# Attention, a routed expert layer and a dense MLP in one kernel: MLP tiles in a new order, rows added up behind each expert, narrower gate products

## The chip, the core and the metric

The kernel runs on one core of one Trainium2 chip. The metric is device time in microseconds (us) of one execution, the median of several. The engines of the core run side by side, each through its own instruction list, and wait for each other through semaphores: TensorE (PE, with its weight loads shown apart as PEld), VectorE (DVE), ScalarE (ACT), GpSimd (POOL) and SyncE (SP, which here only issues DMAs).

## What is computed

Three layers, one behind the other, on 2 x 768 = 1536 tokens of width 512, all in float32:

```python
# 1. attention, 2 x 8 heads of 64, with 4 sink keys and a window of 128
keep = is_sink | in_window
a = softmax(where(keep, q @ k.T / 8, -1e9)); x = a @ v          # -> x: (1536, 512)
# 2. routed experts: tokens with x @ w_skip > 0 go to one of 8 experts
e_idx = argmax(x @ w_gate); gate_w = softmax(x @ w_gate)[e_idx]
out = x.copy()
out[active] = x + gate_w * (relu(x @ w1[e]) @ w2[e])           # w1: (8, 512, 1024)
# 3. dense MLP on every token: 512 -> 2048 -> 512
h = out @ w_in
g = where(h > 0, h, exp(min(h, 0)) - 1)
return g @ w_out
```

With the drawn inputs 653 of the 1536 tokens are active. Their counts by expert are 69, 177, 98, 15, 21, 114, 89 and 70. Of the first 1152 tokens (nine tiles of 128) 561 have no expert.

## The kernel before

**Attention.** Head pairs are worked through in 48 units of 128 queries. TensorE makes the scores (`qk`, line 1280), turns the probabilities (`turn_unit`, 1306), and multiplies by the values (`pv`, 1350). Every second unit it turns the finished columns of `x` (`turn_x`, 1322) and multiplies them by the gate weights (`gate`, 1332). The gate weights `wg` are 9 columns wide (8 experts and the skip score) but stand in a tile of 119 columns, the rest zero (memset in line 663), and the product is made over all 119. The finished rows lie in `x_tok` in SBUF and are stored to `tokens_dram` (line 587).

**Routing** (lines 1121 to 1181 on VectorE, 1421 to 1454 on TensorE). From the scores each active token gets a slot: the experts follow each other in chunks of 128 slots, each expert padded to a whole chunk. Which token stands in which slot is found by small bf16 products: `here` is a 0/1 tile of token against row, made for 12 token tiles, first for chunk 0 alone and then for all chunks; the sums give `sources`, the list of token rows that each chunk gathers. `slot_i` is the reverse: the slot of each token; a token without an expert points past the slots to a row of zeros.

**Experts.** Nine chunks run here (one expert has two). GpSimd gathers a chunk's 128 rows from `tokens_dram` into `xg` by an indirect DMA (`gather_chunk`, lines 696 to 709); the gather of chunk k may start when TensorE has turned chunk k-1 out of `xg` (`xg_turned`). On TensorE a chunk is 64 matrix records of up products (`ps_h`, 1470), the turn of the *next* chunk into `ps_x` (4 records, 1439), and 24 down products (`ps_y`, 1259). ScalarE rounds `h` to its high part (843), copies `ps_x` to `xg_t` (837) and splits the weights to come into high and low halves (476 and 480; the low halves by VectorE, 484 and 489). VectorE copies `ps_y` to `y_sb` (1194), and ScalarE issues its store to `slots_dram` (848).

**From the experts to the MLP.** When the last store has landed, GpSimd gathers the slots of token tiles 0, 1 and 2 into `row_sb` (line 742). VectorE scales each by its gate and adds `x_tok` (`combine`, line 1214). TensorE turns it (1489), ScalarE and VectorE make `x_hi` (868) and `x_lo` (1221), and then the first up product of the MLP may start.

**MLP.** Four blocks of three token tiles, each with 16 steps of 12 up products (`ps_g`, 1259) and 9 down products (`ps_out`, 1514); up products run one step ahead of the activation. The next block's tiles are gathered, combined and turned behind it. SyncE stores `out` tile by tile (637), and GpSimd gathers the next tile into the same buffer after that. SyncE loads the last three weight pieces only behind the first gather of tile 2 (line 630).

The order that matters for the last chunk is, on VectorE and GpSimd:

```python
1192                dve.wait_ge(down_done, g + 2)
...
1194                dve.tensor_copy(y_sb[:], ps_y[:]).then_inc(y_copied, 1)
...
731            pool.wait_ge(y_stored, end * 16 + 16)
...
1213                dve.wait_ge(gathered[i], tb * 16 + 16)
```

Of the kernel before, what the change touches and what calls it, by code (L numbers as in the profile page):

```python
# [16 lines left out]
HOT = 6  # L17
BIG = 3.0e38
# [3 lines left out]
def build(nc, q_t, k_s, v_p, n_sink, window, w_skip, w_gate, w1, w2, w_in, w_out, out):  # L22
# [40 lines left out]
    GW = P - E1  # L63
    DV = DH + 1
    PV = 2 * DV
    assert PC == DC and 2 * DH == P and QT == 2 * PG and 4 * SK == P
# [22 lines left out]
    slots_dram = nc.dram_tensor("slots", [SLOTS + 2 * P, D], F32, kind="Internal").ap()  # L89

    tokens_dram = nc.dram_tensor("tokens", [N + P, D], F32, kind="Internal").ap()
    token_tiles = tokens_dram.rearrange("(t p) d -> p t d", p=P)
    slot_chunks = slots_dram.rearrange("(c p) d -> c p d", p=P)
# [15 lines left out]
    with ExitStack() as ctx:  # L109
# [22 lines left out]
        x_tok = sb("x_tok", [P, NT, D])  # L132
        identity = sb("identity", [P, P])
        gates = sb("gates", [P, NT])
        slot_i = sb("slot_i", [P, NT], I32)
# [9 lines left out]
        with ExitStack() as routing:  # L145
            scope.append(routing)
            wg = sb("wg", [P, DC, GW])
            zeros = sb("zeros", [P, D])
            token_f = sb("token_f", [P, 2, NT])
            scores = sb("scores", [P, NT, E1])  # L150
# [112 lines left out]

        with ExitStack() as experts:
            scope.append(experts)
            xg = sb("xg", [P, D])
# [10 lines left out]
            y_sb = sb("y_sb", [P, D])  # L277
            ps_h = [psum(f"ps_h{i}", [P, KP, P]) for i in range(2)]
            ps_x = psum("ps_x", [P, DC, P])
            ps_y = psum("ps_y", [P, D])  # L280
            ps_source = psum("ps_source", [P, 512])
            scope.pop()


        with ExitStack() as mlp:
            scope.append(mlp)
            x_hi = sb("x_hi", [P, DC, TW], F32R)
            x_lo = sb("x_lo", [P, DC, TW], F32R)
# [7 lines left out]
            row_sb = [sb(f"row_sb{i}", [P, D]) for i in range(TB)]  # L296
            ps_g = [psum(f"ps_g{i}", [P, 512]) for i in range(2)]
            ps_out = [psum(f"ps_out{i}", [P, D]) for i in range(TB)]
            ps_x2 = [psum(f"ps_x2{i}", [P, DC, P]) for i in range(TB)]
# [14 lines left out]
        gate_padded = sem("gate_padded")  # L314
# [62 lines left out]

        xg_loaded = sem("xg_loaded")
# [11 lines left out]
        combined = sem("combined")  # L390
# [140 lines left out]
        def _(sp):  # L531
# [42 lines left out]
            def zero_slots(third):  # L574

                if third == 0:
                    sp.wait_ge(zeros_set, 2)
                    sp.dma_start(tokens_dram[N:, :], zeros[:]).then_inc(tokens_stored, 16)
                every = slots_dram.rearrange("(c p) d -> p c d", p=P)
                first, end = (CHUNKS + 2) * third // 3, (CHUNKS + 2) * (third + 1) // 3  # L580
# [53 lines left out]
            with sp.Fori(0, NB) as tb:  # L634
                for i in range(TB):
                    sp.wait_ge(out_copied, tb * TB + i + 1)
                    sp.dma_start(out_tiles[bass.ds(tb * TB + i, 1)].rearrange("o p d -> (o p) d"),
                                 row_sb[i][:]).then_inc(out_stored[i], 16)
            for i in range(TB):
                sp.wait_ge(out_stored[i], 16 * NB)  # L640

        @block.gpsimd
        def _(pool):
# [19 lines left out]
            pool.memset(wg[:, :, E1:GW], 0.0).then_inc(gate_padded, 1)  # L663
# [8 lines left out]
            iota(chunk_at[:, 0, :], [[P, CHUNKS + 1]])  # L672
            iota(rel[:], [[1, S]], by_partition=-1)
# [3 lines left out]
            pool.wait_ge(iotas_done, 15)  # L677
# [5 lines left out]
            pool.memset(sources[:], N).then_inc(const_done, 1)  # L683
# [12 lines left out]
            def gather_chunk(k):  # L696
                if not (isinstance(k, int) and k == 0):

                    pool.wait_ge(xg_turned, k)
                pool.tensor_copy(source_i[:], sources[:, bass.ds(k, 1)]).then_inc(source_picked, 1)  # L700
                pool.wait_ge(source_picked, k + 1)
                if not (isinstance(k, int) and k == 0):
# [3 lines left out]
                    out=xg[:], out_offset=None, in_=tokens_dram[:, :],  # L706
                    in_offset=bass.IndirectOffsetOnAxis(ap=source_i[:], axis=0),
                    bounds_check=N, oob_is_err=False,
# [8 lines left out]
            gather_chunk(1)  # L717

            for e in range(E):
                first, hi = bases  # L720

                gather_chunk(first + 2)
                with pool.If(first + 1 < hi):
                    with pool.Fori(first + 1, hi) as g:
                        gather_chunk(g + 2)
# [3 lines left out]


            pool.wait_ge(y_stored, end * 16 + 16)
            pool.wait_ge(xg_loaded, end * 16 + 32)
            pool.wait_ge(xg_copied, end + 1)
            pool.wait_ge(idle_done, end + 2)
            pool.tensor_tensor(idle[:], idle[:], idle[:], ALU.subtract).then_inc(idle_done, 1)
            for t in range(NT):

                if t >= 2 * TB:
                    pool.wait_ge(out_stored[t % TB], 16 * (t // TB - 1))
                elif t >= TB:  # L740
                    pool.wait_ge(x2_turned, t - TB + 1)
                pool.indirect_dma_start(
                    out=row_sb[t % TB][:], out_offset=None, in_=slots_dram[:, :],
                    in_offset=bass.IndirectOffsetOnAxis(ap=slot_i[:, t:t + 1], axis=0),
                    bounds_check=SLOTS, oob_is_err=False,
                ).then_inc(gathered[t % TB], 16)

        @block.scalar
        def _(act):
# [89 lines left out]
            def chunk(g, hook):  # L839
                for i in range(2):  # L840
# [6 lines left out]
                act.wait_ge(y_copied, g + 2)  # L847
                act.dma_start(slot_chunks[bass.ds(g, 1)].rearrange("o p d -> (o p) d"),
                              y_sb[:]).then_inc(y_stored, 16)
# [755 lines left out]
```

## Time and profile before

| | us |
|---|---|
| median of 3 runs | 572.84 |
| lowest, highest | 571.85, 573.89 |
| the profiled execution | 572.68 |
| its span, first to last instruction | 570.7 |
| TensorE busy | 536.2 (94%) |
| VectorE, ScalarE, GpSimd busy | 273.4, 211.4, 43.5 |

The stages in the span: attention to about 142, routing to 157, experts to 278, the change-over to 293, the MLP to the end. All times in the text are from the start of the span. In the profile a TensorE record's "busy" holds its latency; how fast a run of products is, is read from the chain or from the distance of two starts. PEclk is the granted TensorE clock as a share of 2.4 GHz: 1.00 is 2.4 and 0.50 is 1.2.

### The profile page before, as it was taken

The page shows a single profiled execution, that of the slowest core. Times are in us where ns is not written, and L with a number is a line of the kernel's source. Part 1 is how long each engine was busy: PE and PEld are TensorE (multiplying, and loading weights), DVE is VectorE, ACT ScalarE, POOL GpSimd, SP SyncE. Part 2 cuts the span into 40 slices and gives each one's busy share as a digit, 9 for nine tenths or more (in the row PEclk, how much of TensorE's full clock was granted, in tenths as well). Part 3 has the DMA queues.
Part 4 walks back from the last instruction along what each step waited for, and adds up shares of the span by engine and source line. Part 5 has one row for each costly group of instructions (what it writes and reads, how often), then busy time and mean ns, then how long its engine had stood idle before and what let it go on. Part 6 is the DMA issues. An engine that isn't in the chain of part 4 may idle for free.

```text
span 570.7 us, 8866 instructions
## 1 busy us (share of the span) xinstructions
PE 536.2 (94%) x3211; PEld 466.3 (82%) x3212; DVE 273.4 (48%) x706; ACT 211.4 (37%) x419; POOL 43.5 (8%) x98
## 2 busy tenths in 40 slices
PE   5999999998599999999579999999999999999997
PEld 3777777777399999999468999898998989999986
DVE  7565655553744144458436663433443344433332
ACT  3575655553033133346214532422233222332222
POOL 6000000000110000100220000010002000000000
PEclk9999999999589999999859999999999999999999
DMA  9288897322029759999472000110003000010001
GB/s 211 73 291 289 262 310 271 113 94 109 23 77 332 259 179 357 354 344 373 152 241 75 2 0 1 57 55 1 0 1 92 18 1 0 0 56 0 1 0 56
DMA packets 47943, 73.21 MB, mean 128 GB/s; under 512 B 16484, under 2 KB 16740, under 8 KB 47908
## 3 DMA queue, kind: packets, MB, share of 16 engines
q1 hardware_dynamic: 43570, 64.23, 33.0%
q0 software_dynamic: 1840, 6.03, 3.5%
q10 hardware_dynamic: 2498, 2.51, 1.3%
q8 instruction: 19, 0.31, 0.2%
q14 instruction: 16, 0.13, 0.1%
HBM read 58.08 MB, written 14.68 MB: 128 GB/s over the span
## 4 chain that ended last, share of the span: by engine, by line
PE 91%; DVE 4%; issue 2%; DMA 2%; ACT 1%; POOL 0%; DVEq 0%; POOLq 0%; ACTq 0%
PE ps_g L1259 24%; PE ps_out L1514 23%; PE ps_h L1470 12%; PE ps_y L1259 9%; PE ps_pv L1350 7%; PE ps_qk L1280 5%; PE ps_turn L1306 4%; PE ps_turn L1332 2%; PE ps_pv L1362 1%; DVE prob L974 1%; PE ps_x L1489 1%; PE ps_x L1439 1%; PE ps_turn L1314 1%; DMA row_sb<-slots,slot_i 1%; DMA xg<-tokens,source_i 1%
## 5 line engine op out<-in xcount | busy, mean ns | idle before, releaser
L1259 PE MATMUL ps_g<-x_hi,w_hi 128*128 128x384 f32 x256 | 87.6, 342 | 1.5 <-DVE x_lo L1221 1.5
L1259 PE MATMUL ps_g<-x_lo,w_hi 128*128 128x384 f32 x256 | 87.1, 340 | 0.0
L1259 PE MATMUL ps_g<-x_hi,w_lo 128*128 128x384 f32 x256 | 87.1, 340 | 0.0
L887 ACT ACTIVATE g_raw<-ps_g 128x384 f32<-128x384 f32 x64 | 31.5, 492 | 129.6 <-PE ps_g L1259 129.5
L1229 DVE TENSOR_SCALAR g_raw<-g_raw 128x384 f32<-128x384 f32 x64 | 23.1, 361 | 116.2 <-ACT g_raw L887 112.0
L1514 PE MATMUL ps_out<-w_hi,g_lo 128*128 128x512 f32 x192 | 75.8, 395 | 0.0
L1514 PE MATMUL ps_out<-w_lo,g_hi 128*128 128x512 f32 x192 | 75.6, 394 | 0.0
L1514 PE MATMUL ps_out<-w_hi,g_hi 128*128 128x512 f32 x192 | 75.5, 393 | 0.0
L1470 PEld LDWEIGHTS ps_h<-xg_t,up_w 128*128 128x128 f32 x576 | 67.7, 197 | 2.0 <-issue 1.3
L1470 PE MATMUL ps_h<-xg_t,up_w 128*128 128x128 f32 x576 | 67.9, 280 | 0.9 <-ACT xg_t L837 0.9
L891 ACT ACTIVATE g_hi<-g_raw 128x384 fp32r<-128x384 f32 x64 | 33.7, 526 | 62.3 <-DVE g_raw L1232 62.3
L1237 DVE TENSOR_TENSOR g_lo<-g_raw,g_hi 128x384 fp32r<-128x384 f32 x64 | 35.7, 558 | 36.1 <-ACT g_hi L891 36.1
L1259 PEld LDWEIGHTS ps_g<-x_hi,w_hi 128*128 128x128 f32 x256 | 49.0, 191 | 4.4 <-issue 1.9
L1259 PEld LDWEIGHTS ps_g<-x_hi,w_lo 128*128 128x128 f32 x256 | 49.0, 191 | 2.6
L1350 PE MATMUL ps_pv<-v_pad,prob_t 128*128 128x130 f32 x352 | 49.5, 282 | 0.0
L1259 PEld LDWEIGHTS ps_g<-x_lo,w_hi 128*128 128x128 f32 x256 | 48.9, 191 | 0.0
L762 ACT ACTIVATE prob<-prob,low 128x288 f32<-128x288 f32 (+1 forms) x96 | 43.6, 504 | 13.5 <-DVE low L974 13.2
L1350 PEld LDWEIGHTS ps_pv<-v_pad,prob_t 128*128 128x128 f32 x352 | 43.7, 193 | 4.2 <-ACT prob_t L776 4.2
L974 DVE CUSTOM_DVE_ANT_0 prob<-ps_qk,bias 128x288 f32<-128x288 f32 (+1 forms) x96 | 38.5, 421 | 13.1 <-PE ps_qk L1280 12.3
L1514 PEld LDWEIGHTS ps_out<-w_hi,g_lo 128*128 128x128 f32 x192 | 36.0, 188 | 8.3
L1514 PEld LDWEIGHTS ps_out<-w_hi,g_hi 128*128 128x128 f32 x192 | 36.0, 188 | 6.2 <-ACT g_hi L891 0.5
L1514 PEld LDWEIGHTS ps_out<-w_lo,g_hi 128*128 128x128 f32 x192 | 36.0, 188 | 6.0
(144 smaller groups left out, 688.0 us busy)
## 6 DMA issues: line engine op xcount, KB each, us to landing
raw<-in_moe_w SPq DMA_DIRECT2D x16, 1024.0 KB, 7.0
up_w<-in_moe_w SPq DMA_DIRECT2D x16, 1024.0 KB
raw<-in_moe_w_in SPq DMA_DIRECT2D x4, 1024.0 KB, 7.1
raw<-in_moe_w_out SPq DMA_DIRECT2D x4, 1024.0 KB, 6.1
slots<-zeros SPq DMA_DIRECT2D x2, 1792.0 KB, 9.5
v_pad<-in_v SPq DMA_DIRECT2D x16, 192.0 KB, 4.8
tokens<-x_tok SPq DMA_DIRECT2D x6, 512.0 KB, 4.5
out_tokens<-row_sb SPq DMA_DIRECT2D x12, 256.0 KB, 2.1
```

The lines of the kernel that those rows point to most:

```text
L762: act.activation(out_, out_, ACT.Exp, bias=low[:, n % 4:n % 4 + 1], scale=-1.0).then_inc(prob_ready, 1)
L887: act.activation(g_raw[f % GB][:], ps_g[f % 2][:, 0:TW], ACT.Exp).then_inc(g_exp_done, 1)
L891: act.activation(g_hi[f % GB][:], g_raw[f % GB][:], ACT.Copy).then_inc(g_hi_done, 1)
L974: dve.tensor_tensor_reduce(out=prob_of(u, h), in0=ps_qk[n % 4][:, 0:w], in1=bias_of(u % QT), scale=-SCALE, scalar=BIG, op0=ALU.add, op1=AL ...
L1229: dve.tensor_scalar(g_raw[f % GB][:], g_raw[f % GB][:], 1.0, 1.0, ALU.min, ALU.subtract).then_inc(g_min_done, 1)
L1237: dve.tensor_tensor(g_lo[f % GB][:], g_raw[f % GB][:], g_hi[f % GB][:], ALU.subtract).then_inc(g_lo_done, 1)
L1259: last = pe.matmul(to, w, x, start=start and m == 0, stop=stop and m == 2)
L1280: pe.matmul(ps_qk[(2 * u + h) % 4][:, 0:w], q_pair[p % 2][rows, i * P:(i + 1) * P], k_pair[p % 2][rows, first:first + w], start=True, stop ...
L1306: last = pe.transpose(ps_turn[h][:, m, :], prob_of(u, h)[:, c:c + P], identity[:])
L1350: last = pe.matmul(ps_pv[g % 2][:, u % 2 * PV:(u % 2 + 1) * PV], prob_t[u % 2][:, h, m, :], v_pad[p % 2][h][:, tile, :], start=(u % 2 == 0 ...
L1470: last = pe.matmul(ps_h[i][:, f, :], up_w[half][i][:, c, f * P:(f + 1) * P], xg_t[:, c, :], start=(c == 0), stop=(c == DC - 1))
L1514: return pe.matmul(ps_out[i][:], act[f % GB][:, i * P:(i + 1) * P], weight, start=(f == 0 and act is g_hi and weight is high), stop=(f == ...
```

## The change

Six things change together.

1. **Order of the MLP.** The tokens of the first nine tiles (`ET` = 9) are sorted: those without an expert first, then by expert. Tiles 9 to 11 keep their order. New work on VectorE (4 operations ahead of the chunk lists, then `place_tokens`: 11 small operations, 9 of 128 columns, 1 copy) and on TensorE (18 products into `ps_place` in the routing, 18 into `ps_list` behind the first expert) makes `lists`: for each place of the nine tiles the row to gather and the row of `out` to write.
2. **One table of rows.** Slots and tokens lie in one DRAM tensor `rows`; a token without an expert is gathered from its token row. The zero rows behind the slots are gone.
3. **Rows are finished in the experts.** ScalarE copies `xg` to `x_keep` (two buffers in turn) behind `xg_t`; VectorE's copy of `ps_y` becomes `ps_y * gate + x_keep`. The gates by slot come from 12 bf16 products of 60 columns (`sum_gates`), which stand behind the first chunk's up products. `combine` is gone, and `x_tok` is no longer kept.
4. **Gathers.** `gather_chunk(k)` waits also for `xg_kept` (the copy to `x_keep`). MLP tile 0 is gathered as if it were one more chunk, and is turned by the last chunk; tiles 1 and 2 are gathered right behind it, without a wait for the last store. ScalarE's store of a chunk moves to the start of the next chunk.
5. **First up product.** The 8 products with `x_hi` run first, before the wait for `x_lo`. Output tiles 0 to 8 are written by GpSimd's indirect DMAs.
6. **Gate products** are 9 columns wide, not 119; the memset of the padding goes.

The core of the diff:

```diff
-                last = pe.matmul(ps_gate[:, i * E1:i * E1 + GW], xt_sb[:, i, :],
+                last = pe.matmul(ps_gate[:, i * E1:(i + 1) * E1], xt_sb[:, i, :],
...
 def gather_chunk(k):
         pool.wait_ge(xg_turned, k)
+        pool.wait_ge(xg_kept, k)
+        pool.wait_ge(y_stored, (k + FREE - TB * 2) * 16)
...
-            pool.wait_ge(y_stored, end * 16 + 16)
-            pool.wait_ge(xg_loaded, end * 16 + 32)
-            pool.wait_ge(xg_copied, end + 1)
-            pool.wait_ge(idle_done, end + 2)
+            for t in range(1, TB):
+                gather_tile(t)
+            pool.wait_ge(y_stored, (end + FREE) * 16)
+            pool.wait_ge(idle_done, end + 1)
             pool.tensor_tensor(idle[:], idle[:], idle[:], ALU.subtract)
-            for t in range(NT):
...
+            for i in range(TB):
+                if i:
+                    pool.wait_ge(x2_turned, i)
+                gather_tile(TB + i)
...
 def turn_in(g):   # ScalarE
                 act.activation(xg_t[:], ps_x[:], ACT.Copy).then_inc(xg_copied, 1)
+                act.activation(x_keep[:, bass.ds(g % 2, 1), :]..., xg[:], ACT.Copy).then_inc(xg_kept, 1)
...
 # VectorE, routing, between the first and the second lists
+            ordered(dve.tensor_tensor(in_class[:], hot_b[:, 0:ET, :], class_e[:]..., ALU.mult))
+            ordered(dve.tensor_reduce(class_of[:]..., in_class[:], AX_X, ALU.add))
+            ordered(dve.tensor_tensor(member[:], class_no[:]..., class_of[:]..., ALU.is_equal))
+            ordered(dve.tensor_tensor(lower[:], class_no[:]..., class_of[:]..., ALU.is_gt))
...
 def chunk(g, hook, first=False):   # VectorE
-                dve.tensor_copy(y_sb[:], ps_y[:]).then_inc(y_copied, 1)
+                dve.wait_ge(xg_kept, g + 1)
+                dve.scalar_tensor_tensor(out=y_sb[:], in0=ps_y[:], scalar=gate_slot[:, bass.ds(g, 1)],
+                                         in1=x_keep[:, bass.ds(g % 2, 1), :]...,
+                                         op0=ALU.mult, op1=ALU.add).then_inc(y_copied, 1)
...
 # TensorE
+            def sum_gates():
+                pe.wait_ge(gates_named, 1)
+                for t in range(NT):
+                    last = pe.matmul(ps_gates[:, 0:3 * CHUNKS], here[:, t, :], gates_as[:, :, t, :],
+                                     start=(t == 0), stop=(t == NT - 1))
...
+            chunk(0, 0, 0, first=True)     # up products, sum_gates, turn, down products
...
+            for t in range(ET):
+                pe.wait_ge(there_ready, t + 1)
+                for m in range(2):
+                    last = pe.matmul(ps_list, there[:, t, :], listed_as[:, m, t]...,
+                                     start=(t == 0 and m == 0), stop=(t == ET - 1 and m == 1))
...
             def turn_tile(tb, i):
-                pe.wait_ge(combined, tb * TB + i + 1)
+                pe.wait_ge(gathered[i], (tb + (1 if i else 0)) * 16)
...
+                if isinstance(tb, int) and tb == 0 and f == 0:
+                    pe.wait_ge(x2_hi_done, TB)
+                    ...                       # 8 products with x_hi
+                    pe.wait_ge(x2_lo_done, TB)
+                    ...                       # 4 products with x_lo
...
-            for i in range(TB):
+            for i in range(1, TB):
                 turn_tile(0, i)
```

## Rows read from the trace of the kernel before

**Rows 1.** The page's 40 slices of the span (14.3 us each): granted TensorE clock.

```profile
PEclk9999999999589999999859999999999999999999
```

**Rows 2.** Chain of waits at the change-over: start us, us, what it is.

```profile
272.25 0.44 PE ps_x L1439 x4
272.69 5.59 PE ps_y L1259 x24
...
279.25 2.01 DMA slots<-y_sb
...
292.63 6.99 PE ps_g L1259 x24
299.62 2.08 PE ps_out L1514 x9
301.71 2.10 PE ps_g L1259 x12
```

**Rows 3.** Stretches: us, busy (x instructions) of each engine, PEclk, DMA share, GB/s.

```profile
278.30:290.00 11.70, 2.23 (x8) 1.43 (x8) 2.98 (x5) 1.03 (x2) 4.21 (x5) 0.62 0.26 90
292.60:296.00 3.40, 3.37 (x11) 3.40 (x12) 0.00 (x0) 0.00 (x0) 0.33 (x1) 0.50 0.97 317
```

**Rows 4.** Timeline around the change-over: start us, us, engine, line, operation [idle before].

```profile
278.40 0.69 DVE L1194 COPY y_sb<-ps_y 128x512 f32<-128x512 f32 x1 [1.90 <-PE ps_y L1259]
...
289.88 1.28 DVE L1221 TENSOR_TENSOR x_lo<-ps_x,x_hi 128x512 fp32r<-128x512 f32 x2
...
291.17 0.60 ACT L868 ACTIVATE x_hi<-ps_x 128x512 fp32r<-128x512 f32 x1 [1.00 <-PE ps_x L1489]
...
296.85 0.49 ACT L887 ACTIVATE g_raw<-ps_g 128x384 f32<-128x384 f32 x1 [5.08 <-PE ps_g L1259]
...
298.36 0.53 ACT L891 ACTIVATE g_hi<-g_raw 128x384 fp32r<-128x384 f32 x1 [1.02 <-DVE g_raw L1232]
```

**Rows 5.** Timeline of the expert stage, the turn of a chunk and the next gather.

```profile
219.38 0.60 PE L1439 MATMUL ps_x<-identity,xg 128*128 128x128 f32 x4
...
221.11 1.04 POOL L705 DMA_INDIRECT xg<-tokens,source_i  x1 [0.50 <-issue]
...
221.97 0.59 ACT L837 ACTIVATE xg_t<-ps_x 128x512 f32<-128x512 f32 x1
...
232.54 0.60 PE L1439 MATMUL ps_x<-identity,xg 128*128 128x128 f32 x4
```

**Rows 6.** All gathers of chunks (line 705): time from issue to landing.

```profile
DMA to landing us min/median/max: 3.4/5.9/6.6
```

**Rows 7.** All gathers of MLP tiles (line 742): the same.

```profile
DMA to landing us min/median/max: 3.7/4.3/8.3
```

**Rows 8.** Timeline of ScalarE in the last two experts.

```profile
261.48 0.58 ACT L837 ACTIVATE xg_t<-ps_x 128x512 f32<-128x512 f32 x1
...
266.69 1.06 ACT L476 ACTIVATE w_hi<-raw 128x1024 fp32r<-128x1024 f32 x1 [2.73 <-DMA raw<-in_moe_w_out]
```

**Rows 9.** Timeline of the routing and the start of the first chunk.

```profile
143.45 0.26 DVE L1126 TENSOR_TENSOR t_a<-scores,top 128x96 f32<-128x96 f32 x1
...
143.75 0.26 DVE L1129 SCALAR_TENSOR_TENSOR hot<-t_a,rank_e 128x96 f32<-128x96 f32 x1
...
145.31 0.64 PE L1428 MATMUL ps_rank<-hot_b,ones 128*128 128x88 bf16 x11
...
152.54 2.29 PE L1452 MATMUL ps_source<-named,here 128*128 128x20 bf16 x24 [2.64 <-DVE here L1172]
...
155.38 1.12 PE L1439 MATMUL ps_x<-identity,xg 128*128 128x128 f32 x4 [0.55 <-DMA xg<-tokens,source_i]
```

**Rows 10.** Chain of waits in attention: a run of products as x records.

```profile
137.74 0.44 PE ps_turn L1332 x4
138.18 0.91 PE ps_pv L1350 x8
139.09 0.44 PE ps_pv L1362 x2
```

More of the change, by code:

```diff
@@ L17 @@
 HOT = 6
+CLASSED = 4
 BIG = 3.0e38
@@ L1180, in _, with chunk @@
             dve.wait_ge(routed, 1)
-            dve.wait_ge(list_step, 9)
-            def chunk(g, hook):
+            def chunk(g, hook, first=False):
                 for i in range(2):
@@ L1241, in mlp_block @@
                         (lo_second if second else lo_first)(dve, n)
-                    if not last and FT - 8 <= f < FT - 8 + TB:
-                        combine(tb + 1, f - (FT - 8))
-            for i in range(TB):
-                combine(0, i)
             low_rows(0)
@@ new lines, in sum_gates, with chunk @@
+            def sum_gates():
[3 more added lines that the diff above has]
+                                     start=(t == 0), stop=(t == NT - 1))
+                last.then_inc(gates_summed, 1)
+            def chunk(pair, half, g, first=False):
+                at = DOWN_AT[half]
+                pe.wait_ge(xg_copied, g + 1)
+                pe.wait_ge(up_loaded[half], pair * (16 * NP) + 16 * NP)
+                for i in range(2):
+                    for f in range(KP):
+                        for c in range(DC):
+                            last = pe.matmul(ps_h[i][:, f, :], up_w[half][i][:, c, f * P:(f + 1) * P],
+                                             xg_t[:, c, :], start=(c == 0), stop=(c == DC - 1))
+                    last.then_inc(up_done, 1)
+                if first:
+                    sum_gates()
+                turn(g + 1)
+                pe.wait_ge(y_copied, g + 1)
+                for i in range(2):
+                    piece_ready(pair * (2 * NP) + half * NP + i)
+                    pe.wait_ge(h_lo_done, g * 2 + i + 1)
+                    for f in range(KP):
+                        last = three(ps_y[:], (h_hi[i][:, f, :], h_lo[i][:, f, :]),
+                                     (w_hi[at + i][:, f, :], w_lo[at + i][:, f, :]),
+                                     i == 0 and f == 0, i == 1 and f == KP - 1)
+                last.then_inc(down_done, 1)
@@ new lines, in expert @@
+            def expert(pair, half):
+                lo, hi = [pe.value_load(base_i[0:1, bass.ds(pair * 2 + half + m, 1)], min_val=0, max_val=CHUNKS - 1 + m)
+                          for m in range(2)]
+                with pe.Fori(lo, hi) as g:
+                    chunk(pair, half, g)
+            chunk(0, 0, 0, first=True)
+            second = pe.value_load(base_i[0:1, 1:2], min_val=1, max_val=CHUNKS - E + 1)
+            with pe.If(second > 1):
+                with pe.Fori(1, second) as g:
+                    chunk(0, 0, g)
@@ new lines, in _ @@
+            for t in range(ET):
+                pe.wait_ge(there_ready, t + 1)
+                for m in range(2):
+                    last = pe.matmul(ps_list, there[:, t, :], listed_as[:, m, t].rearrange("p k j -> p (k j)"),
+                                     start=(t == 0 and m == 0), stop=(t == ET - 1 and m == 1))
+            last.then_inc(lists_summed, 1)
+            expert(0, 1)
+            with pe.Fori(1, E // 2) as pair:
+                for half in range(2):
+                    expert(pair, half)
@@ L1496, in up @@
                     piece_ready(NPX + 2 * m)
+                if isinstance(tb, int) and tb == 0 and f == 0:
+                    pe.wait_ge(x2_hi_done, TB)
+                    for c in range(DC):
+                        for half in (w_hi, w_lo):
+                            pe.matmul(ps_g[0][:, 0:TW], half[MLP_AT[0]][:, c, 0:P], x_hi[:, c, :],
+                                      start=(c == 0 and half is w_hi), stop=False)
+                    pe.wait_ge(x2_lo_done, TB)
+                    for c in range(DC):
+                        last = pe.matmul(ps_g[0][:, 0:TW], w_hi[MLP_AT[0]][:, c, 0:P], x_lo[:, c, :],
+                                         start=False, stop=(c == DC - 1))
+                    last.then_inc(g_up_done, 1)
+                    return
                 if f == 0:
```

274 lines of the change are left out of this document (184 added, 90 removed).

## The prediction, made before the changed kernel was run

> **What bounds the kernel now.** I read four views. First the page's slices of the granted clock [rows 1]: TensorE runs at 2.4 GHz in 35 of the 40 slices. Two of the dips lie in the routing, two at the change-over from the experts to the MLP, the last in the final slice. There TensorE had stood still and then worked for a while at 1.2 GHz. Everywhere else the engine is the bound: the experts are a gapless series of 64 up records, 4 turns and 24 down products, and the MLP one of 12 and 9 products, 2.1 us each [rows 2]. Second, the chain of waits at the change-over. The last down product ends at 272.69 + 5.59 = 278.28, the first MLP product starts at 292.63, and the first down product of the MLP at 299.62 [rows 2]. So 21.3 us pass for 24 products that cost 4.2 us at full clock (12 cost 2.10). Third, the stretches: from 278.3 to 290.0 TensorE is busy 2.2 of 11.7 us, and the clock is 0.50 in 292.6 to 296.0 [rows 3]. The 24 products take 6.99 us for that reason, 2.8 us more than at 2.4 GHz. Fourth, the timeline, for what the wait is made of: a copy of `ps_y`, a store of 2.01 us, gathers, a combine, a turn, `x_hi` and `x_lo` [rows 2, 4].
>
> **The change-over, step by step.** I keep the times of before until 278.28.
> - Of the old line store, gather, combine nothing is left ahead of the first product, provided that the three tiles are there. Tile 0 is turned by the last chunk (the 4 records at 272.25 [rows 2], which today turn an unused chunk, so they cost nothing new). Tiles 1 and 2 are 8 records of 0.11 us: 0.9 us, to 279.2.
> - ScalarE: `x_hi` of tile 0 is done before 278; those of tiles 1 and 2 take 0.60 each [rows 4] behind the turns, the last until about 279.95. TensorE waits 0.8 us for it, and starts at 280.0.
> - 8 products with `x_hi`: 1.4 us, to 281.4. Meanwhile VectorE finishes `y_sb` (from 278.40; 0.69 as a copy, here with a second input, I take 0.75) and makes three `x_lo` at 1.28 / 2 = 0.64 each [rows 4], to 281.1. That is 0.3 us before they are wanted, so splitting the product hides them. 4 products with `x_lo`: to 282.1.
> - The second up product ends at 284.2. The first down product wants `g_hi`: from the exponential's start to the end of `g_hi` it is 298.36 + 0.53 - 296.85 = 2.04 us [rows 4], and the exponential starts some 0.2 us behind the up product. So it starts at 284.4, against 299.62: 15.2 us less. The missing 2.8 us of slow clock are in that number, since TensorE now rests for under 1 us at a time. From there on the MLP is bound by TensorE as before.
>
> **Are the tiles there?** Of the first 1152 tokens 561 have no expert, so tiles 0 to 2 (384 rows) hold only token rows, which were stored long ago; the wait on `y_stored` asks for a third chunk only. In time: the copy to `x_keep` follows `xg_t` (261.48 + 0.58 [rows 8]) and takes about the same, to 262.7. GpSimd's steps between its release and the gather were 1.1 us (219.98 to 221.11 [rows 5]), so the gather of tile 0 is issued at 263.8. The slowest chunk gather landed 6.6 us after issue [rows 6]: 270.4, wanted at 272.25 [rows 2]. Tiles 1 and 2 are issued some 1.3 us apart behind it (an issue is 1.04 [rows 5]), the last at 266.4. The slowest tile gather took 8.3 [rows 7]: 274.7, wanted at 278.1. On ScalarE the store of chunk 7 now stands behind the split that waits for a weight piece until 266.69 [rows 8]; only the last `y_sb` waits for that store, 9 us later.
>
> **The other chunks.** The gather of each chunk is now released by the copy to `x_keep`, not by the turn: 221.97 + 0.59 + 0.6 = 223.2, and the issue moves from 221.11 to about 224.2. With 6.6 us it lands at 230.8, and the turn is at 232.54 [rows 5, 6]. I take it at nothing, with 1.7 us of cover. Two more things stand in line on ScalarE behind `xg_t`: 0.6 us per chunk, where only the two experts before the MLP have more than two pieces to split. VectorE's `y_sb` grows by under 0.1 us and is wanted 7 us later.
>
> **What is added on TensorE's path.**
> - Routing: four small VectorE operations ahead of the second lists. Two neighbours of that size start 0.30 apart (143.45 and 143.75 [rows 9]), so they cost 1.2 us. The second lists end at 154.8 and the first turn starts at 155.38, held by its gather [rows 9]; 0.6 of the 1.2 us is covered. Cost 0.6. The 18 `ps_place` products (1.0 us at the price below) fit into the 2.64 us for which TensorE waits for `here`. `place_tokens` on VectorE, about 5 us, lies under the first up products (9 us), and delays its first `h_lo` by nothing that TensorE sees.
> - `sum_gates`, 12 products, and the 18 of `ps_list`. The nearest row is `ps_rank`: 11 bf16 products in 0.64 us, 0.058 each, at 1.2 GHz [rows 9]. At 2.4 GHz the price is between half of that and all of it: 0.35 to 0.7 and 0.5 to 1.05. Semaphore waits stand between the 18, so I take the upper half: 0.5 and 0.8.
> - GpSimd's stores of `out` and its gathers in the MLP have a block of some 67 us (16 steps of 4.2) to be done. Free. The last three stores stay SyncE's.
>
> **The gate products.** They go from 119 to 9 columns; 24 gates with 4 records each, 96 records. A run of 4 takes 0.44 us, 0.110 each; products of 130 columns take 0.91 / 8 = 0.114; those of 260 columns 0.22 [rows 10]. By columns alone 119 would be 0.101. So something else, the load of 128 weight columns by all likelihood, already sets 0.110, and it does not get shorter. I take 0; the ends are 0 and 96 x 0.1 = 9 us of gain, if it were the columns.
> On this the Trainium skill has two rules, both in "TensorE: Matmul & The Clock Gate". Its section "Back-to-back issue gap" lets the distance of two products shrink with the columns, down to a floor; the section "LDWEIGHTS (loading the stationary operand)" gives a weight load of 128 columns 128 / 1.2 = 107 ns, whatever is multiplied. The 0.110 of rows 10 at 119 columns agrees with the second. By the first the sum below would be some 8 us lower, by the second it stays.
>
> **Sum.** -15.2 + 0.6 + 0.5 + 0.8 = -13.3 us. The profiled execution took 572.68 (span 570.7 and 2.0 around it); the median of the runs is 572.84, 0.16 above, less than the runs differ among themselves. Forecast: 572.7 - 13.3 = 559.4 us. Own range 557.5 to 561.5: the bf16 prices give -0.5 to +0.5, the change-over and the point at which the clock rises in the first chunk another 1.5 either way.
>
> **Rivals.**
> - *Clock.* The padded gate products, or the short turns at the change-over, may have kept the clock up. Of the 24 gates 20 stand in attention's full row of work, and for the change-over a rest of under 1 us speaks against it: the clock fell only behind standstills of several us [rows 1, 3]. But the last four gates, from 136 us on, stand where TensorE has little else. Price: each fall costs what it cost at the change-over, 2.8 us; one to three falls: 562 to 568. Chance 0.12.
> - *Columns count.* The gates shorten by up to 96 x 0.085 = 8 us, partly taken by waits for VectorE: 551 to 557. Against it: rows 10. Chance 0.07.
> - *Gathers late, and slower than before.* The gather now starts 3.1 us later in each chunk, when the up weights are loading. TensorE waits from a landing of 232.54 - 224.2 = 8.3 us on, in seven chunks, and from 8.3 + 13.3 / 7 = 10.2 us on the kernel is slower than before. At 10.5 us it gives 559.4 + 7 x 2.2 = 575. Against it: no chunk gather took over 6.6 [rows 6]. Chance 0.03. A milder case, 9 us, gives 564: chance 0.05.
> - *It doesn't do what it says.* Tiles 1 and 2 are not in by 278.1, for instance because the weight pieces fill the DMA queues, and TensorE stands and cools again: up to 4 us of wait and 2.8 us of clock, 566. Chance 0.04, since 8.3 us would still leave 3.
>
> **Chances.** Forecast 0.69, clock 0.12, columns 0.07, gathers mildly late 0.05, tiles late 0.04, slower 0.03. To leave out no more than 2 in 10 the range goes from 556.5 to 565.5: without the columns, the slower case and the ends of the others. A measurement of this kernel can tell 0.3%, 1.7 us, from no change. All cases but the last are faster than that; 0.01 of the milder gather case I give to no change. Faster 0.96, same 0.01, slower 0.03.
>
> **What would show it.** In the profile after: the chain at the change-over holds no DMA, and from the last `ps_y` to the first `ps_out` pass 6.1 us; the granted clock is 1.00 from the first chunk to the end, without the dip at the change-over; the turns of the chunks follow the up products without a wait for `xg`; the first chunk starts 0.6 us later; a run of 4 gate records still takes 0.44 us in attention. The forecast is wrong if the attention stage ends at another time than 142, or if a chunk takes other than 13.2 us.

## The result and the profile after

The changed kernel takes 559.45 us (median of four executions, 558.8 to 560.5), the kernel before 572.38 beside it. The ratio is 0.9773, with a 95% interval of 0.9755 to 0.9791. The forecast was 559.4 us. The profiled execution took 558.8 us with a span of 557.0, against 572.7 and 570.7: 13.7 us of span less, where the forecast had 13.3; between the medians it is 12.9.

So the number came out. What must be asked is whether it came out by the terms of the sum. The first view is the page's granted clock, beside [rows 1]: the dip at the change-over is gone, that of the routing is there as before.

```profile
PEclk9999999999679999999999999999999999999999
```

The chain of waits at the change-over (start us, us, what), beside [rows 2]:

```profile
275.16 5.59 PE ps_y L1379 x24
280.75 0.45 PE ps_x L1643 x4
...
281.71 0.60 ACT x_hi L937
282.31 0.14 issue
282.45 1.64 PE ps_g L1655 x8
284.09 0.70 PE ps_g L1659 x4
284.79 2.08 PE ps_g L1379 x12
...
287.01 2.31 PE ps_out L1680 x9
```

Lines 1655 and 1659 are the 8 products with `x_hi` and the 4 with `x_lo` of the first up product. No DMA stands in the chain. From the end of the last `ps_y` (280.75) to the first `ps_out` (287.01) pass 6.26 us, against 21.34 before. The chain at the first chunk:

```profile
156.59 9.34 PE ps_h L1600 x64
165.93 0.33 PE ps_gates L1589 x12
166.25 0.47 PE ps_x L1558 x4
166.73 5.60 PE ps_y L1379 x24
172.33 0.35 PE ps_x L1631 x14
...
173.39 0.26 PE ps_x L1631 x4
...
175.02 7.38 PE ps_h L1600 x64
```

The products of line 1631 are those of `ps_list`, which the trace shows under the name `ps_x`. The 12 products for the gates cost 0.33 us, the lower price of the forecast, but from the end of the first chunk's down products (172.33) to the next up product (175.02) pass 2.69 us, for 18 tiny products. Before, these two followed each other without a gap:

```profile
167.29 5.61 PE ps_y L1259 x24
172.90 7.14 PE ps_h L1470 x64
```

TensorE's waits between 160 and 290 us (engine, line, waited for: us, times, longest) name no engine and no DMA for it (the second row belongs to the change-over):

```profile
PE ps_h L1600 <- issue: 1.4, 1, 1.4
PE ps_g L1655 <- ACT x_hi L937: 0.8, 1, 0.8
PE ps_x L1631 <- issue: 0.7, 1, 0.7
```

By the borders that these chains give, the two profiled executions differ as follows. The borders are the `scores` behind the last gate, the first `ps_h`, the start of what follows the first chunk's down products, the first `ps_h` of the second chunk, the end of the last `ps_y` and the first `ps_out`.

| stage | before | after | difference | forecast |
|---|---|---|---|---|
| attention, to the last `scores` | 142.36 | 141.35 | -1.0 | 0 |
| routing, to the first `ps_h` | 15.02 | 15.24 | +0.2 | +0.6 |
| first chunk | 15.52 | 15.74 | +0.2 | +0.5 |
| behind the first chunk (`ps_list`) | 0 | 2.69 | +2.7 | +0.8 |
| the other chunks | 105.38 | 105.73 | +0.35 | 0 |
| change-over | 21.34 | 6.26 | -15.1 | -15.2 |
| MLP, from the first `ps_out` to the end | 271.1 | 270.0 | -1.1 | 0 |
| sum | 570.7 | 557.0 | -13.7 | -13.3 |

The large term is right. The small ones are not: 1.9 us too little for `ps_list`, and two gains of 1 us that no step had. Of the 0.35 in the other chunks 0.24 stand right behind `ps_list`, in the second chunk's up products (7.38 instead of 7.14).

### The profile page after: what moved, and what is told of

Read it like the earlier page. It is cut to its first block, busy times and chain, and to the rows that moved or that the text cites. A ratio compares the mean times of both kernels' runs of the same rounds, so it can differ in the third digit from the quotient of the medians.

```text
span 557.0 us, 8962 instructions
## 1 busy us (share of the span) xinstructions
PE 531.4 (95%) x3255; PEld 462.9 (83%) x3256; DVE 273.3 (49%) x726; ACT 216.5 (39%) x429; POOL 49.9 (9%) x108
## 4 chain that ended last, share of the span: by engine, by line
PE 93%; DVE 4%; issue 2%; ACT 1%; DVEq 0%
PE ps_out L1680 24%; PE ps_g L1379 24%; PE ps_h L1600 12%; PE ps_y L1379 9%; PE ps_pv L1469 7%; PE ps_qk L1400 5%; PE ps_turn L1425 4%; PE ps_turn L1451 2%; PE ps_pv L1481 1%; DVE prob L1045 1%; PE ps_x L1558 1%; PE ps_turn L1441 1%; PE ps_turn L1433 1%; PE ps_x L1643 1%; PE ps_source L1564 0%
## 5 line engine op out<-in xcount | busy, mean ns | idle before, releaser
L1379 PE MATMUL ps_g<-x_hi,w_hi 128*128 128x384 f32 x252 | 85.0, 337 | 0.0
L1379 PE MATMUL ps_g<-x_lo,w_hi 128*128 128x384 f32 x252 | 84.7, 336 | 0.0
L1379 PE MATMUL ps_g<-x_hi,w_lo 128*128 128x384 f32 x252 | 84.6, 336 | 0.0
L1379 PEld LDWEIGHTS ps_g<-x_hi,w_lo 128*128 128x128 f32 x252 | 47.3, 188 | 2.4
L1379 PEld LDWEIGHTS ps_g<-x_hi,w_hi 128*128 128x128 f32 x252 | 47.3, 188 | 2.4
L1379 PEld LDWEIGHTS ps_g<-x_lo,w_hi 128*128 128x128 f32 x252 | 47.3, 188 | 0.0
L1045 DVE CUSTOM_DVE_ANT_0 prob<-ps_qk,bias 128x288 f32<-128x288 f32 (+1 forms) x96 | 38.5, 421 | 12.9 <-PE ps_qk L1400 12.1
```

The source lines that it names most:

```text
L1045: dve.tensor_tensor_reduce(out=prob_of(u, h), in0=ps_qk[n % 4][:, 0:w], in1=bias_of(u % QT), scale=-SCALE, scalar=BIG, op0=ALU.add, op1=AL ...
L1379: last = pe.matmul(to, w, x, start=start and m == 0, stop=stop and m == 2)
```

## Was the change-over won by the order, and what part of it was the clock?

First, the clock alone, in the kernel before.

```diff
+            piece_ready(NPX)
+            busy(34)           # ps_source <- w_hi, 512 columns
             for i in range(TB):
                 turn_tile(0, i)
+                busy((2, 4, 7)[i])
             up(0, 0, True)
```

> The kernel before, with TensorE kept busy at the change-over: 34 products of 512 columns that nobody reads while the store and the gathers run, then 2, 4 and 7 behind the turns of the three tiles. The order of the change-over is untouched. Theory (the 24 products in 6.99 us were slow through the clock): the granted clock stays at 1.00 and they take 4.2 us, the kernel is 2.8 us faster, 569.6 us. Rival (they were slow because the DMA queues were 0.97 full or for the first reading of new weights): they still take 6 to 7 us and the time is 572.4 or above. If the filler ends behind the last turn, up to 1 us of the gain is lost.

Measured: 569.44 us against 572.03, ratio 0.9951 (0.9936 to 0.9967). The chain:

```profile
292.84 4.31 PE ps_g L1259 x24
...
297.29 2.31 PE ps_out L1514 x9
```

The same 24 products that took 6.99 us in [rows 2] take 4.31; the nine behind them take 2.31 instead of 2.08, and the kernel gained 2.6. The DMA engines are as full as before in this stretch (share 1.00 against 0.97 [rows 3]), and only the granted clock differs, 1.00 against 0.50. So 2.7 of the 15.1 us are the clock, as the forecast had it (2.8), and at the same full queues these products are not slow.

Then the order, in the kernel after (on ScalarE the store stands ahead of `high_rows(0)` besides).

```diff
-            for t in range(1, TB):
-                gather_tile(t)
             pool.wait_ge(y_stored, (end + FREE) * 16)
             ...
+            for t in range(1, TB):
+                gather_tile(t)
```

> The kernel after, except that the gathers of MLP tiles 1 and 2 wait for the last store of y rows as the kernel before did, and that ScalarE issues this store ahead of its splits of x; tile 0 and everything else stay in the new order. Theory (the gain of the change-over is that no MLP row waits for a store): from the last ps_y to the first ps_out 18 to 21 us instead of 6.3, the first 24 products back at 6 to 7 us with the clock at 0.5, and 12 to 15 us are lost: 571 to 574 us. Rival (the gain came from the combine that was taken out and from tile 0 being in early): TensorE waits only for one gather behind the store, 6 to 8 us lost, 566 to 568 us.

Measured: 571.84 us, 12 more than the kernel after; the ratio to the kernel before is 1.0000 (0.9985 to 1.0014). The profiled execution was the shortest of eight (568.8), and in it the change-over took 296.90 - 280.20 = 16.7 us:

```profile
281.54 2.03 DMA rows<-y_sb
...
285.78 3.29 DMA row_sb<-rows,lists
...
291.01 2.90 PE ps_g L1655 x8
```

The expected length, 18 to 21 us, was too long: the combine is gone here and one wait, of 7.5 us, serves both tiles. So in this execution 10.4 of the 15.1 us come from the order itself, 1.3 of them through the clock (the first 12 products take 3.7 us instead of 2.3). The other 4.6 (21.3 - 16.7) are what still sets this chain apart from the old one: tile 0 in early, no combine, the split of the first product, and the first 24 products in 5.8 us instead of 7.0. No run takes these apart. By this edit alone the store and the gather of the old chain are back, and in the median of the runs the whole gain of the change is gone.

Last, the split of the first up product, for which the forecast had 0.3 us of distance.

```diff
                     pe.wait_ge(x2_hi_done, TB)
+                    pe.wait_ge(x2_lo_done, TB)
                     for c in range(DC):
                     ...
-                    pe.wait_ge(x2_lo_done, TB)
```

> The kernel after, with the first MLP up product waiting for all x_lo before it starts, as before the change. In the trace after the last x_lo ends at 283.71 and the 8 products with x_hi started at 282.45. Theory: splitting the product hides this, so without it the start moves to about 283.8 and the kernel loses 1.2 to 1.4 us (1.0023 of the kernel after). Rival (the forecast had x_lo 0.3 us ahead of its need, but with so small a distance another wait may be the last): 0.3 us or less.

Measured: 562.01 us, 2.0 above the kernel after beside it (560.06) and 2.6 above its first median. The start moved by what was expected, from 1.70 to 3.11 us behind the last `ps_y`. As much again is the clock: from the last `ps_y` to the first `ps_out` pass 9.1 us instead of 6.26, of which 1.4 are the later start and 1.4 the slower products. These are the chain, and two stretches with the busy time of PE, PEld, DVE, ACT, POOL and then the clock, DMA share and GB/s:

```profile
283.37 2.90 PE ps_g L1656 x8
286.27 0.89 PE ps_g L1659 x4
```

```profile
283.30:285.00 1.70, 1.63 (x5) 1.66 (x6) 0.00 (x0) 0.00 (x0) 0.00 (x0) 0.50 0.99 369
...
287.20:289.00 1.80, 1.80 (x12) 1.74 (x10) 0.92 (x2) 0.78 (x2) 1.08 (x2) 1.00 0.00 0
```

With 2.2 us of rest instead of 0.8 the clock fell to 1.2 GHz and the 12 products cost 3.8 instead of 2.3 us. In this chain the split is worth 2.9 us, twice what the wait alone says; the medians, which scatter, have 2.0 to 2.6.

## Where the 2.7 us behind the first chunk come from

The 18 products themselves are 0.35 + 0.26 us, about the lower price of the forecast. The rest is called "issue": 0.70 us ahead of the last four products and 1.37 behind them. For the 0.70 the trace has no record, and in two other runs with this gap (the ones with the late gathers of tiles 1 and 2, and with 64 bytes of room) it is missing and the gap 1.46 us; its cause stays open. For the 1.37 there is one. The trace's records of TensorE's sequencer show what it does there: behind the first of the last four products two loads from the table `base_i` (0.31 us at 173.41, 0.30 at 174.07) with their register steps, until 174.9. They are the loop bounds of the next expert. In the kernel before, the same loads stand at 168.8 to 170.4, under the first chunk's down products, where the sequencer runs ahead of the long products. To test it the sums were moved to where long products follow.

```diff
                 if first:
                     sum_gates()
+                    sum_lists()        # e4: the 18 products of ps_list here
...
                 for i in range(2):
+                    if first and i == 1:
+                        sum_lists()    # e5: or here
```

> The kernel after, unchanged, beside the next three on the same chip. Expected: 0.977 of before, 559 us.

Measured: 560.06 us, ratio 0.9781 (0.9749 to 0.9813).

> The kernel after, with the 18 products of ps_list moved from behind the first chunk into it, behind the 12 of ps_gates. Theory (the 2.7 us between the last down product of chunk 0 and the first up product of chunk 1 are mostly TensorE's instruction stream: the value loads and the branch of the next expert are no longer read ahead under the down products, and the short products drain the queue): 1.4 us of issue and 0.7 us between the short products go, 0.5 us of products stay: 2.0 us less, 0.9965 of the kernel after. Rival (the branches of the first expert, which the change wrote out, cost the same wherever the short products stand): 0 to 0.4 us less.

Measured: 557.86 us, ratio to before 0.9755 (0.9733 to 0.9777), 2.2 us less than the kernel after beside it.

```profile
166.70 0.33 PE ps_gates L1589 x12
167.03 0.44 PE ps_x L1597 x18
167.47 0.49 PE ps_x L1558 x4
167.97 5.60 PE ps_y L1379 x24
173.56 7.14 PE ps_h L1608 x64
```

> The kernel after, with the 18 products of ps_list between the first and the second 12 down products of chunk 0. By the theory of the run before: again 2.0 us less than the kernel after, since 12 long products (2.8 us) follow under which the value loads can be read ahead. Rival: 0 to 0.4 us less.

Measured: 557.79 us, ratio 0.9739 (0.9715 to 0.9764).

```profile
171.63 0.45 PE ps_x L1597 x18
172.08 2.90 PE ps_y L1379 x12
174.98 7.15 PE ps_h L1608 x64
```

At both places the 18 products cost 0.44 to 0.45 us and the second chunk follows without a gap. The loads and the branches are in both kernels too, so it is their place behind short products that costs, not their number. The intervals of these ratios overlap that of the kernel after, and three of its six executions (557.3 to 558.7) are as short as these; the gap that is gone in the chain is the firmer evidence.

The second profiled execution of the kernel after shows one cause of its scatter by 5 us (557.3 to 562.2), worth 1.5 us. In it the second chunk's up products took 8.91 us, not 7.38 (chain), and the granted clock at their start (third number from the right) was 0.52, not 1.00:

```profile
176.25 8.91 PE ps_h L1600 x64
```

```profile
176.20:179.60 3.40, 3.35 (x16) 3.38 (x17) 0.00 (x0) 0.00 (x0) 0.00 (x0) 0.52 0.96 322
```

```profile
175.00:178.40 3.40, 3.38 (x30) 3.40 (x31) 0.00 (x0) 0.00 (x0) 0.00 (x0) 1.00 1.00 309
```

The first stretch is of that execution, the second of the one above: after the same gap the clock had fallen in the one and not in the other. The four other profiled runs with products of `ps_list` at this place have 7.38 us. The scatter of the six executions goes with the mean granted clock: the three of 561.5 to 562.2 us have 0.977 to 0.981, the three of 557.3 to 558.7 have 0.984 and 0.985. Where the clock fell in the executions without a profile is not shown.

## The gate products

```diff
-    GW = P - E1
+    GW = E1
...
-            pool.memset(wg[:, :, E1:GW], 0.0).then_inc(gate_padded, 1)
...
-                pe.wait_ge(gate_padded, 1)
```

> The kernel before with one part of the change alone: the gate products have 9 columns instead of 119 (no zeros, no wait for them). Theory: all that attention gained comes from here. A run of 4 gate records takes 0.35 us as after the change, not 0.44, about 0.1 us less in each of 24 gates, of which some lies beside waits: routing begins 1.0 us earlier and the kernel is 1.0 us faster, 571.4 us. Rival (the forecast's price of nothing: the load of the weights sets the time of a product): the run stays at 0.44 and the time at 572.4.

Measured: 571.62 against 572.03 us, ratio 0.9993 (0.9981 to 1.0004). The interval reaches from 1.1 us less to 0.2 more, so the time alone can't tell the theory's 1.0 us from nothing. The record of a gate did get shorter, as the theory had it, but see the chain of the kernel after around one gate, beside [rows 10]:

```profile
136.87 0.35 PE ps_turn L1451 x4
137.22 1.00 PE ps_pv L1469 x8
138.22 0.44 PE ps_pv L1481 x2
```

The run of four took 0.44 and takes 0.35; the eight products behind it took 0.91 and take 1.00. Together 1.35 us both times. The narrow products start sooner one after the other, and the next ones wait for it. Only where TensorE has to wait behind a gate is something left, as behind the last one (first the kernel before, then after):

```profile
27.44 0.70 PE L1332 MATMUL ps_turn<-wg,xt_sb 128*128 128x119 f32 x4
...
141.61 0.70 PE L1332 MATMUL ps_turn<-wg,xt_sb 128*128 128x119 f32 x4 [0.47 <-ACT xt_sb L784]
```

```profile
26.95 0.61 PE L1451 MATMUL ps_turn<-wg,xt_sb 128*128 128x9 f32 x4
...
140.70 0.61 PE L1451 MATMUL ps_turn<-wg,xt_sb 128*128 128x9 f32 x4 [0.47 <-ACT xt_sb L846]
```

From the first gate to the last it is 141.61 - 27.44 = 114.17 us with 119 columns and 140.70 - 26.95 = 113.75 with 9. This distance is the same within 0.04 us in every profiled kernel of either kind; the first gate's start is not, it lies anywhere between 26.76 and 28.29. With the 0.09 of the last gate the narrow products are worth 0.5 us, and the other 0.5 of the table's -1.0 is the scatter of the start. The Trainium skill has in "TensorE: Matmul & The Clock Gate", section "LDWEIGHTS (loading the stationary operand)", that a weight load of 128 columns takes its time, 107 ns, whatever is multiplied. The sum of 1.35 us for 12 products, 0.113 each, agrees with it nearly; the run of four alone, 0.35 / 4 = 0.088 each, does not.

## How much room the gathers had

```diff
-                act.activation(xg_t[:], ps_x[:], ACT.Copy).then_inc(xg_copied, 1)
+                for n in range(2):
+                    act.activation(xg_t[:], ps_x[:], ACT.Copy).then_inc(copied_once, 1)
+                    act.wait_ge(copied_once, g * 2 + n + 1)
+                act.activation(xg_t[:], ps_x[:], ACT.Copy).then_inc(xg_copied, 1)
```

> The kernel after, but ScalarE copies xg_t three times in a row, so that x_keep, and with it the release of the next gather, come some 1.3 us later in each chunk. The xg_t copies themselves have 4 us until TensorE wants them. Theory (in the trace after the rows of chunks 5 to 8 come in only 0.4, 0.5, 0.9 and 0.5 us ahead of their turns, of the others 2 us and more): TensorE waits 0.9, 0.8, 0.4 and 0.8 us before these turns, the kernel is 2.5 to 3.5 us slower than after the change, 562 to 563 us. Rival (the forecast's cover of 1.7 us holds): no wait before a turn and no loss beyond 0.3 us.

Measured: 562.57 us (ratio to before 0.9849, 0.9824 to 0.9874), about 3 us more than the kernel after. TensorE's waits between 160 and 290 us, and the longest wait in the chain:

```profile
PE ps_x L1562 <- DMA xg<-rows,source_i: 2.2, 2, 1.7
```

```profile
244.31 7.56 DMA xg<-rows,source_i
...
251.92 0.66 PE ps_x L1562 x4
```

The total was as expected (2.5 to 3.5), its parts only half so: two waits of 2.2 us in all instead of four, and 0.9 us in the first chunk, where two more copies stand ahead of the first up product, which the expectation had left out. In any case a gather released 1.3 us later (6.3 us behind its turn, as 244.31 to 238.04, and not 5.0, as 240.02 to 235.02) arrives late. In the kernel after the row beside [rows 6] is:

```profile
DMA to landing us min/median/max: 3.4/7.3/8.2
```

From an issue to the next turn it is 8.2 us (240.02 to 248.21). The forecast had 8.3 for that, rightly, but set 6.6 against it, the slowest landing of the kernel before. The slowest is 8.2 now. The cover was not 1.7 us but, for the slowest, nothing to be spoken of: the gather issued at 213.57 landed at 221.76, 0.04 us ahead of its turn. Why the gathers land later in the new place was not tested.

## The MLP's 1.1 us

In every kernel with the new order so far the stretch from the start of the first `ps_out` to the end of the last takes 266.7 us, in every one with the old 267.7 to 267.8. First suspected were the PSUM banks.

```diff
+            ps_x2 = [psum(f"ps_x2{i}", [P, DC, P]) for i in range(TB)]
             ps_g = [psum(f"ps_g{i}", [P, 512]) for i in range(2)]
             ps_out = [psum(f"ps_out{i}", [P, D]) for i in range(TB)]
-            ps_x2 = [psum(f"ps_x2{i}", [P, DC, P]) for i in range(TB)]
```

> The kernel before with one thing of the change that no step of the forecast costs: the PSUM banks of the MLP are given out in the order of the kernel after (the three banks of the turns first, then those of ps_g and of ps_out). In every kernel with the new order the time from the first ps_out to the last is 266.7 us, in every one with the old 267.7 to 267.8. Theory: the banks set it; 266.7 us and the kernel 1.0 us faster, 0.9982 of before. Rival: it comes with something else of the change (MLP gathers and stores, another queue): 267.7 us and the time unchanged.

Measured: 572.39 us, ratio 1.0004 (0.9992 to 1.0015), the stretch 267.8 us. It isn't this order of the banks. Another thing that differs is the addresses of the tiles in SBUF.

```diff
+        room = sb("room", [P, 80])     # e10, in before; [P, 16] in after for e11
         identity = sb("identity", [P, P])
```

> The kernel before with 320 unused bytes per partition in SBUF ahead of the weight slots 4 to 7, g_hi, g_lo and what is allotted between them. With that these tiles start at the same address modulo 2048 as in the kernel after. No instruction is changed. Theory (the 1.05 us that the MLP gained between its first and last ps_out come from where its operands lie in SBUF): a run of 9 down products takes 2.067 us as after the change, not 2.086, the stretch 266.7 us, not 267.7, and the kernel is 1.0 us faster, 0.998 of before. Rival (it comes with other work that the change moved, such as the MLP's gathers): 2.086 and 267.7 us, the time unchanged.

Measured: ratio 1.0002 (0.9993 to 1.0012), the stretch 267.9 us. The nine down products took 2.082 us instead of 2.086, the twelve up products 2.099 instead of 2.093: the times of the runs changed, but there was no gain.

> The kernel after with 64 unused bytes per partition at the same place, so that its tiles behind it start at the same address modulo 256 as in the kernel before. Theory of the run before, with a distance as small as this deciding it: the run of 9 down products goes back to 2.086 us and the stretch to 267.7 us, 1.0 us slower than the kernel after. Rival (addresses don't matter, or only in larger steps): 2.067 and 266.7 us.

Measured: 559.97 us, which the scatter of the kernel after doesn't tell from it; but the stretch is 268.4 us, 1.7 more than in every other kernel with the new order, and the nine down products take 2.093 us on average instead of 2.067. The direction is the expected one, the size (1.0 us, 2.086) is not. The stretch from 300 to 540 us fits it by the number of TensorE's products, for the kernel before, the kernel after, and the last two in turn:

```profile
300.00:540.00 240.00, 240.00 (x1223) 217.22 (x1222) 104.65 (x197) 73.64 (x140) 6.03 (x6) 1.00 0.07 21
```

```profile
300.00:540.00 240.00, 240.00 (x1229) 218.22 (x1228) 95.36 (x185) 70.87 (x137) 15.20 (x15) 1.00 0.05 17
```

```profile
300.00:540.00 240.00, 240.00 (x1221) 217.44 (x1221) 104.54 (x196) 73.85 (x140) 6.05 (x6) 1.00 0.06 21
```

```profile
300.00:540.00 240.00, 240.00 (x1220) 217.00 (x1220) 94.72 (x185) 70.60 (x136) 15.18 (x15) 1.00 0.05 17
```

TensorE is busy all the time and the clock is 1.00 in all four, and yet 1229, 1223, 1221 or 1220 products fit. Shown is that 64 bytes of room, with no instruction changed, cost the MLP 1.7 us. That the addresses also explain the 1.1 us between before and after is not shown: the expectation that equal addresses modulo 2048 bring it failed. Other things that the change moved in the MLP, its gathers and stores, were not tested. Which operands must lie how stays open.

## A version that beats both

The routing still has its cold stretch, and the first chunk pays for it. The last experiment keeps TensorE busy there, on top of the version with `ps_list` behind `ps_gates`.

```diff
+            busy(11, ps_rank)          # bf16, 512 columns of ones, read by nobody
             pe.wait_ge(route_step, HOT)
...
+            busy(5, ps_y)
...                                     # before each pair of products of a list:
+                busy(1, ps_y, 2)       # 256 columns
...
+            busy(4, ps_y)
             pe.wait_ge(order_step, CLASSED)
...
+            busy(8, ps_y)
             pe.wait_ge(first_named, 1)
```

> The version with ps_list summed behind ps_gates (557.9 us), and TensorE kept busy through the routing: 11, 5, 4 and 8 bf16 products of 512 columns that nobody reads where it stood still, and one of 256 columns between any two products of the slot lists. Theory (the clock falls at the standstill behind the last gate, and the first chunk pays for it: 64 up products in 9.3 to 10.1 us instead of 7.14, the first turn in 0.97 instead of 0.45): the clock stays at 1.00, and 2.7 us go, 555.2 us. Rival (bf16 products against a weight of ones, or gaps that are left, don't keep the clock): the up products still take over 9 us, and the filler delays the lists by 0 to 1 us: 557.9 to 559 us.

Measured: 554.27 us (554.09 to 556.21), ratio to before 0.9694 (0.9679 to 0.9708), 18 us faster than the kernel before.

```profile
155.28 0.53 PE ps_x L1565 x4
...
156.49 7.41 PE ps_h L1619 x64
```

```profile
PEclk9999999999999999999999999999999999999999
```

The first turn takes 0.53 us instead of 0.97, the up products 7.41 instead of 9.34 to 10.1, and the mean granted clock of the execution is 1.00. The gain on the version with `ps_list` behind `ps_gates` (557.86) is 3.6 us, where 2.7 were expected; the two were measured beside different runs of the kernel before, and by their ratios it is 3.5.

## Why the prediction was right, step by step

- *Change-over, -15.2.* Right: -15.1, with the order worth 10.4 in the profiled execution of the run that put the store back in front, and the clock 2.7 by the run with filler. Its inner steps held to 0.2 us: the first product started 1.70 us behind the last `ps_y` (forecast 1.7), the last `x_lo` ended at 283.71, 0.4 us before it was wanted (0.3), and the first `ps_out` came after 6.26 us (6.1).
- *Routing, +0.6.* It was 0.2. The four operations took 1.1 us (1.2 in the forecast), of which 0.55 fell into the wait for the first gather [rows 9], as in the forecast; the rest is that the first turn took 0.97 us and not 1.12, and that the first up product followed `xg_t` after 0.04 us and not 0.24.
- *`sum_gates`, +0.5.* 0.33 us; that is the lower price, 0.028 us each, half of [rows 9]. The first chunk grew by 0.2 only, since its up products took 9.34 us and not 9.47.
- *`ps_list`, +0.8.* The mis-sized term: 2.7. At the two other places that were tried the same products cost 0.45. The step "so many products by so much" left out what the sequencer does behind them, and 0.7 us between them that stay unexplained. A row for it stood in the trace of before, among the sequencer's records, but no view of the chain shows it while long products hide it.
- *Gates, 0.* Nearly right in its size: 0.5 us, in places where TensorE waits. Its reason held for the sum of 12 products and not for the run of four, which did get shorter. The rival "columns count", with up to 8 us, is refuted by the run that has nothing else.
- *Gathers, 0 with 1.7 us of cover.* The time was right, the cover wrong. The milder rival, late gathers, begins at a landing of 8.3 us, and the slowest took 8.2. It had been given 0.05 on the argument that no gather took over 6.6 us, and that was not so in the new place.
- *Clock falls elsewhere.* That rival was half right: not behind the gates, but behind `ps_list`, where the clock fell in one of the two profiled executions of the kernel after and cost 1.5 us.
- *MLP, unchanged.* It was 1.1 us faster, through something no step looked at.
- *The signs.* The chain without a DMA, the 6.1 us, the missing dip and the turns without a wait came out. Three did not: the run of four gate products took 0.35 us and not 0.44, attention ended at 141.35 and not 142 (half of it is the scatter of its start), and the first chunk, which should begin 0.6 us later, began 0.8 us earlier, 0.2 later counted from the last gate. The granted clock was 1.00 only from 160.7 us on, some 4 us into the first chunk, where before it was 161.7.
- *A reading.* [rows 1] shows 36 slices with a 9 and four below, not 35 and five; the last slice is no dip (granted clock 1.00 from 556.4 to 570.7). No term of the sum rests on it.

So 559.4 was met in part by luck, since errors cancelled: +1.9 for `ps_list` and +0.35 in the chunks against -0.3 and -0.4 in the first chunk and the routing, -1.0 in attention and -1.1 in the MLP. The range held it for the right reason, the size of the change-over.

## What to carry to other kernels

Take the store of the last rows out of the path of the first ones: where most rows of a table don't depend on the last stage, sort these first, and the wait of store, gather and combine goes away whole, as it did here with the slow clock behind it. Don't put a run of tiny products right ahead of a stretch of the instruction list with loads and branches: here it cost 2.7 us, and 0.45 ahead of long products, under which the sequencer could read on. And don't take the slowest landing of the old place for a gather that is moved: here the median went from 5.9 to 7.3 us and the slowest from 6.6 to 8.2.

## What was not expected of the hardware

- In the profiled executions a rest of TensorE of 0.8 us did not lower its clock and one of 2.2 us did. The gap of 1.5 to 2.7 us with 18 tiny products in it did so in one of six.
- Products that nobody reads keep the clock up: 28 of 512 columns and 24 of 256 in the routing save more than they cost, 3.6 us in all.
- A run of four fp32 products of 9 columns takes 0.35 us instead of 0.44, and the next eight products give the 0.09 us back.
- Unused room of 64 bytes in SBUF made nine down products take 2.093 us instead of 2.067 and the MLP 1.7 us longer, with TensorE fully busy both times.
